# First group's sums in eight PSUM banks and two passes, its late rows from three queues, GpSimd's long products in quarters

## The reference, cut to what matters

```python
u = x * v
h = (np.maximum(pos_emb @ w1, 0) @ w2) * np.exp(-0.01 * pos)[:, None]
y = np.fft.irfft(np.fft.rfft(u, n=2 * S, axis=1) * np.fft.rfft(h, n=2 * S, axis=0), n=2 * S, axis=1)[:, :S]
a = x * y                                            # long convolution, gated
b = np.maximum(a @ w_in, 0) ** 2 @ w_out             # layer 1, 2048 hidden units
h = b @ w_in2
out = (np.maximum(h, 0) + alpha * np.minimum(h, 0)) @ w_out2   # layer 2
```

## Time and profile before

| | |
|---|---|
| median of 3 runs | 1471.96 us (1470.58 to 1472.6) |
| the profiled execution | 1473.5 us |
| its span | 1471.7 us |
| PE busy | 1451.9 us (99%) |
| DVE, ACT, POOL busy | 965.4, 799.9, 69.6 us |
| mean granted clock of PE | 0.992 |

### The profile page before, as it was taken

One profiled execution on the slowest core, in us unless ns is written; L12 is line 12 of the kernel. 1 busy time (PEld: TensorE's weight loads), 2 busy tenths in 40 slices (PEclk: granted clock), 3 DMA queues, 4 the chain that ended last, 5 costly groups with the idle time before them and its releaser, 6 DMA issues.

```text
span 1471.7 us, 18934 instructions
## 1 busy us (share of the span) xinstructions
PE 1451.9 (99%) x7106; PEld 1267.4 (86%) x7106; DVE 965.4 (66%) x1075; ACT 799.9 (54%) x1034; POOL 69.6 (5%) x51
## 2 busy tenths in 40 slices
PE   8999999799999999999999999999999999999998
PEld 8998888789888888888888888888888888888887
DVE  6876666466666666666666666666666666666664
ACT  3776677434554555455555555555555555555553
POOL 4500011121000000000000000000000000000000
PEclk9999999889999999999999999999999999999999
DMA  9545977451011011100000000000000000000000
GB/s 253 176 147 164 305 231 238 143 164 45 22 29 29 1 29 29 29 8 7 7 7 0 7 7 7 7 7 7 0 7 7 7 7 7 7 0 7 7 8 14
DMA packets 47446, 80.17 MB, mean 54 GB/s; under 512 B 4620, under 2 KB 29426, under 8 KB 46626
## 3 DMA queue, kind: packets, MB, share of 16 engines
q1 hardware_dynamic: 45170, 69.49, 15.8%
q10 hardware_dynamic: 2224, 9.98, 2.0%
HBM read 60.14 MB, written 19.23 MB: 54 GB/s over the span
## 4 chain that ended last, share of the span: by engine, by line
PE 97%; DVE 1%; ACT 1%; DMA 1%; SPq 0%; issue 0%; DVEq 0%; ACTq 0%
PE ps L172 12%; PE ps L174 12%; PE ps L161 12%; PE ps L162 12%; PE ps L173 12%; PE ps L163 12%; PE ps L627 5%; PE ps L593 4%; PE ps L672 4%; PE ps L616 3%; PE ps L608 3%; PE ps L601 1%; PE ps L576 1%; DVE g_lo L353 1%; PE ps L153 0%; PE ps L154 0%
## 5 line engine op out<-in xcount | busy, mean ns | idle before, releaser
L330 DVE SCALAR_TENSOR_TENSOR g<-ps,relu 128x960 f32<-128x960 f32 x208 | 240.7, 1157 | 199.0 <-ACT relu L278 195.9
L278 ACT ACTIVATE relu<-ps 128x960 f32<-128x960 f32 x208 | 202.6, 974 | 300.5 <-PE ps L163 300.5
L353 DVE TENSOR_TENSOR g_lo<-g,g_hi 128x960 fp32r<-128x960 f32 x208 | 245.5, 1180 | 168.7 <-ACT g_hi L291 168.6
L291 ACT CAST g_hi<-g 128x960 fp32r<-128x960 f32 x208 | 207.1, 996 | 236.1 <-DVE g L330 236.1
L172 PE MATMUL ps<-g_hi,w_hi 128*128 128x480 f32 x832 | 320.6, 385 | 3.0 <-DVE g_lo L353 2.0
L174 PE MATMUL ps<-g_lo,w_hi 128*128 128x480 f32 x832 | 319.1, 384 | 0.0
L162 PE MATMUL ps<-x_hi,w_lo 128*128 128x480 f32 x832 | 316.5, 380 | 0.0
L173 PE MATMUL ps<-g_hi,w_lo 128*128 128x480 f32 x832 | 316.3, 380 | 0.0
L161 PE MATMUL ps<-x_hi,w_hi 128*128 128x480 f32 x832 | 316.1, 380 | 0.1
L163 PE MATMUL ps<-x_lo,w_hi 128*128 128x480 f32 x832 | 313.2, 376 | 0.0
L362 DVE SCALAR_TENSOR_TENSOR g_lo<-ps,g_hi 128x960 fp32r<-128x960 f32 x208 | 239.3, 1150 | 12.9 <-ACT g_hi L298 12.9
(11 more groups left out here) (54 smaller groups left out, 1009.9 us busy)
## 6 DMA issues: line engine op xcount, KB each, us to landing
work<-dft_back SPq DMA_DIRECT2D x49, 256.0 KB, 2.9
g_dram<-work SPq DMA_DIRECT2D x49, 256.0 KB, 3.3
gt<-g_dram SPq DMA_DIRECT2D x14, 784.0 KB
gt<-x_seq SPq DMA_DIRECT2D x32, 196.0 KB
work<-v_seq SPq DMA_DIRECT2D x32, 196.0 KB
work<-dft_forward SPq DMA_DIRECT2D x49, 128.0 KB, 3.4
x<-x_gate ACTq DMA_DIRECT2D x4, 1560.0 KB, 8.1
out_t<-x SPq DMA_DIRECT2D x26, 240.0 KB, 2.0
```

The lines of the kernel that those rows point to most:

```text
L278: nc.scalar.activation(relu1[:], h[0][:, :, :T], ACT.Relu).then_inc(relu1_ready, 1)
L291: nc.scalar.copy(g_hi[0][:, s // 2 % 2], g1[:]).then_inc(g1_hi_ready, 1)
L330: nc.vector.scalar_tensor_tensor(out=g1[:], in0=h[0][:, :, :T], scalar=0.0, in1=relu1[:], op0=ALU.max, op1=ALU.mult).then_inc(g1_ready, 1)
L353: nc.vector.tensor_tensor(g_lo[0][:, s // 2 % 2], g1[:], g_hi[0][:, s // 2 % 2].bitcast(FP32), ALU.subtract).then_inc(g1_lo_ready, 1)
```

## The change

It has three parts. (1) Group 0's sums go over all eight banks, one for each of its 4 x 2 columns: a first pass over the real rows, a second over the imaginary rows, blk 1 first; the banks 7 and 6 come last in the first pass, since ACT still copies from them. The real rows of groups 0 and 1 are loaded at k = 29 and 32, the older imaginary ones at k = 42 and 43, the rest at k = 48. (2) The moves of the last two steps' rows are issued by three engines: SP takes the first half of a step (`i` = 0), ACT the second (`i` = 1), and GpSimd all four moves of step 47 for group 1, under a semaphore of their own. (3) GpSimd's three long products are cut into four pieces each, and those who wait for one now wait for four pieces.

```diff
@@ feed_forward
             if chunks[0] == 0:
-                pe.wait_ge(w_alpha_ready, 1)
+                pe.wait_ge(w_alpha_ready, F // (4 * P))
...
-                                pe.wait_ge(w3_lo_ready, 1)
+                                pe.wait_ge(w3_lo_ready, F // (4 * P))
...
         def round_0():
-            for m in range(ROUND_0):
+            sum_first_group(pe)
+            for m in range(2, ROUND_0):
                 sum_half(pe, m)
...
-                        act.wait_ge(w_scaled, 1)
+                        act.wait_ge(w_scaled, F // (4 * P))
...
-        nc.gpsimd.tensor_tensor(w_alpha.rearrange("p (c d) -> p c d", d=P),
-                                w_raw[3].rearrange("p (c d) -> p c d", d=P),
-                                alpha_sb[:].unsqueeze(2).to_broadcast([P, F // P, P]),
-                                ALU.mult).then_inc(w_alpha_ready, 1)
-        pool.wait_ge(w_alpha_ready, 1)
-        nc.gpsimd.tensor_tensor(w_raw[3], w_raw[3], w_alpha, ALU.subtract).then_inc(w_scaled, 1)
-        pool.wait_ge(w3_hi_ready, 1)
-        nc.gpsimd.tensor_tensor(w_lo[3][:], w_raw[3], w_hi[3][:].bitcast(FP32), ALU.subtract).then_inc(w3_lo_ready, 1)
+        for c in range(0, F // P, 4):
+            nc.gpsimd.tensor_tensor(w_alpha.rearrange("p (c d) -> p c d", d=P)[:, c:c + 4],
+                                    w_raw[3].rearrange("p (c d) -> p c d", d=P)[:, c:c + 4],
+                                    alpha_sb[:, c:c + 4].unsqueeze(2).to_broadcast([P, 4, P]),
+                                    ALU.mult).then_inc(w_alpha_ready, 1)
+        parts = [slice(c, c + 4 * P) for c in range(0, F, 4 * P)]
+        for n, at in enumerate(parts):
+            pool.wait_ge(w_alpha_ready, n + 1)
+            nc.gpsimd.tensor_tensor(w_raw[3][:, at], w_raw[3][:, at], w_alpha[:, at], ALU.subtract).then_inc(w_scaled, 1)
+        for n, at in enumerate(parts):
+            pool.wait_ge(w3_hi_ready, 1)
+            nc.gpsimd.tensor_tensor(w_lo[3][:, at], w_raw[3][:, at], w_hi[3][:, at].bitcast(FP32),
+                                    ALU.subtract).then_inc(w3_lo_ready, 1)
...
+        gate_half(dve, 1)
         gate_half(dve, 0)
-        gate_half(dve, 1)
         split_x1(0)
@@ long_convolution
-    def load_rows(sp, q, half, rows):
+    def load_rows(sp, q, half, rows, loaded):
...
+    moved_by_pool = sem("moved_by_pool")
+
+    def move_rows(engine, q, k, i, moved):
+
+        for part in range(2):
+            row, first = 2 * (2 * k + i) + part - R, N1 * part + GN * q
+            engine.dma_start(gt_buffers[q][row:row + 1, 1], g_sb[first:first + GN, k % 3, i]
+                             ).then_inc(moved, 16)
+
+    EARLY = K_STEPS - 8
+    early_rows = [slice(0, 2 * (2 * EARLY) - R), slice(2 * (2 * EARLY) - R, 2 * (2 * (K_STEPS - DIRECT)) - R)]
...
-                if k == EARLY + 1:
-                    stored(sp, EARLY)
-                    for q in range(2):
-                        load_rows(sp, q, 0, slice(0, R))
-                        load_rows(sp, q, 1, early_rows[0])
+                for q in range(2):
+                    if k == K_STEPS // 2 + 5 + 3 * q:
+                        stored(sp, K_STEPS // 2 + 1)
+                        load_rows(sp, q, 0, slice(0, R), half_0_loaded[q])
+                    if k == EARLY + 1 + q:
+                        stored(sp, EARLY)
+                        load_rows(sp, q, 1, early_rows[0], half_1_loaded[q])
+                sp.wait_ge(g_copied, k)
+                for q in range(k + DIRECT - K_STEPS):
+                    move_rows(sp, q, k - 1, 0, half_1_loaded[q])
                 if k == K_STEPS - DIRECT + 1:
                     stored(sp, K_STEPS - DIRECT)
                     for q in range(2):
-                        load_rows(sp, q, 1, slice(early_rows[0].stop, early_rows[1].stop))
-                sp.wait_ge(g_copied, k)
-                if k > K_STEPS - DIRECT:
-                    move_rows(sp, 0, k - 1)
+                        load_rows(sp, q, 1, early_rows[1], half_1_loaded[q])
                 sp.dma_start(g_dram[4 * k - 4:4 * k]...
...
+        pool.wait_ge(g_copied, K_STEPS - 1)
+        for i in range(2):
+            move_rows(pool, 1, K_STEPS - DIRECT, i, moved_by_pool)
...
+    def sum_first_group(pe):
+
+        def sums(banks, half):
+            for bank in banks:
+                blk, n = divmod(bank, GN)
+                if half == 0 and bank >= 6:
+                    pe.wait_ge(g_copied, K_STEPS - bank % 2)
+                last = nc.tensor.matmul(ps[:, bank, :R], gt_buffers[0][:R, half, n, blk * P:(blk + 1) * P],
+                                        idft98_sb[:R, half], start=half == 0, stop=half == 1)
+            return last
+
+        pe.wait_ge(idft98_loaded, 16)
+        pe.wait_ge(half_0_loaded[0], 16)
+        sums((0, 1, 2, 3, 4, 5, 7, 6), 0)
+        pe.wait_ge(half_1_loaded[0], 16 * (2 + 8))
+        sums(range(GN, 2 * GN), 1).then_inc(last_done, 1)
+        sums(range(GN), 1).then_inc(last_done, 1)
+
     def sum_half(pe, h):
...
-        if blk == 0 and q < 2:
-            pe.wait_ge(early_loaded[q], 16 * EARLY_DMAS)
+        if h == 2:
+            pe.wait_ge(half_0_loaded[1], 16)
+            pe.wait_ge(half_1_loaded[1], 16 * (2 + 4))
+            pe.wait_ge(moved_by_pool, 16 * 4)
...
     def gate_half(dve, h):
...
-        y = ps[:, 6 + h % 2, :GN * R].rearrange("p (n m) -> p m n", m=R)[:, :rows, :]
+        dve.wait_ge(last_done, h + 1 if h >= 2 else 2 - h)
+        if h < 2:
+            y = ps[:, GN * h:GN * (h + 1), :rows].rearrange("p n m -> p m n")
+        else:
+            y = ps[:, 6 + h % 2, :GN * R].rearrange("p (n m) -> p m n", m=R)[:, :rows, :]
...
     def scalar_program(act):      # result_copy(k)
-                move_rows(act, 1, k)
+                for q in range(k + 1 + DIRECT - K_STEPS):
+                    move_rows(act, q, k, 1, half_1_loaded[q])
```

More of the change, by code:

```diff
@@ L69, in feed_forward @@
     acc = [ps[:, 4 + k, :] for k in range(2)]
-    sum_half, gate_half, load_group, last_done, gated, w_hi_ready, w_lo_ready, alpha_loaded = last_stage
+    sum_first_group, sum_half, gate_half, load_group, last_done, gated, w_hi_ready, w_lo_ready, alpha_loaded = last_stage
     PIECES = 12
@@ L466, in long_convolution @@
     w_hi_ready, w_lo_ready = sem("w_hi_ready"), sem("w_lo_ready")
-    early_loaded = [sem(f"early_loaded{q}") for q in range(2)]
+    half_0_loaded, half_1_loaded = ([sem(f"half_{half}_loaded{q}") for q in range(2)] for half in range(2))
     gt_loaded = [sem(f"gt_loaded{b}") for b in range(3)]
@@ L481, in stored @@
             engine.wait_ge(g_stored[b], 16 * len(range(b, steps, 3)))
-    def load_rows(sp, q, half, rows):
[L485 to L497, removed]
+    def load_rows(sp, q, half, rows, loaded):
+        sp.dma_start(gt_buffers[q][rows, half], g_halves[rows, half, GN * q:GN * (q + 1), :]).then_inc(loaded, 16)
+    moved_by_pool = sem("moved_by_pool")
[6 more added lines that the diff above has]
+    early_rows = [slice(0, 2 * (2 * EARLY) - R), slice(2 * (2 * EARLY) - R, 2 * (2 * (K_STEPS - DIRECT)) - R)]
     def load_group(sp, q):
@@ L657, in tensor_program @@
                 inverse(k - 1)
+    def sum_first_group(pe):
[13 more added lines that the diff above has]
+        sums(range(GN), 1).then_inc(last_done, 1)
     def sum_half(pe, h):
         q, blk = h // 2, h % 2
-        if h == 0:
-            pe.wait_ge(g_copied, K_STEPS)
-            pe.wait_ge(idft98_loaded, 16)
         b = BUFFER[q]
-        if blk == 0 and q < 2:
-            pe.wait_ge(early_loaded[q], 16 * EARLY_DMAS)
+        if h == 2:
+            pe.wait_ge(half_0_loaded[1], 16)
+            pe.wait_ge(half_1_loaded[1], 16 * (2 + 4))
+            pe.wait_ge(moved_by_pool, 16 * 4)
         elif blk == 0:
             pe.wait_ge(gt_loaded[b], 16 * BUFFER[2:q + 1].count(b))
-        wait(pe, gated, h - 1)
+        pe.wait_ge(gated, h - 1)
         for n in range(GN):
@@ L679, in gate_half @@
         rows = size // GN
-        dve.wait_ge(last_done, h + 1)
-        if h == 0:
+        if h == 1:
             for k in range(4):
                 dve.wait_ge(gate_loaded[k], 16)
-        y = ps[:, 6 + h % 2, :GN * R].rearrange("p (n m) -> p m n", m=R)[:, :rows, :]
+        dve.wait_ge(last_done, h + 1 if h >= 2 else 2 - h)
[3 more added lines that the diff above has]
+            y = ps[:, 6 + h % 2, :GN * R].rearrange("p (n m) -> p m n", m=R)[:, :rows, :]
         x = x1[:, first:first + size].rearrange("p (m n) -> p m n", n=GN)
@@ L819, in long_convolution @@
     programs = sync_program, tensor_program, scalar_program, vector_program, gpsimd_program
-    return programs, (sum_half, gate_half, load_group, last_done, gated, w_hi_ready, w_lo_ready, alpha_loaded)
+    return programs, (sum_first_group, sum_half, gate_half, load_group, last_done, gated, w_hi_ready, w_lo_ready, alpha_loaded)
 def token_order(S):
```

## The result

The changed kernel takes 1462.49 us (median of 4 runs, 1461.83 to 1465.0), the kernel before 1472.28 (4 runs, 1470.58 to 1475.22): ratio 0.9935, 95% interval 0.9915 to 0.9954. That is 9.8 us less, inside the range of 1456 to 1466.8, but 4.5 us above the 1458 that was called likeliest, and where rival B stood (1461.6 to 1463.3). The profiled execution took 1465.0 us, its span is 1462.2.

A forecast was written before the change was run, and what follows sets the result against it. PE was taken as the bound, busy 1451.9 of 1471.7 us. Half 4 12.3 us earlier plus 2.0 of `g_lo` waits made 14.3: 1473.5 to 1459.2 profiled, median 1.5 lower, so 1458; range 1456 to 1466.8.

The forecast's parts named there:

- rival B: Clock falls in the 1.3 us idle time ahead of the second pass, 1463.3, or only after that pass, 1461.6; chance 0.24.
- A: Everything as summed, with the clock staying up through group 0's and 1's sums: 1458 us; chance 0.45.
- So I take the clock as staying up: Between the two passes PE idles 1.3 us, yet the sums behind run at full clock; half 4 12.3 us earlier.
- The moves: Last rows' moves issued by three engines: second pass can start at 282.0 instead of 285.52; bounds 281.6 and 282.9.
- GpSimd's moves: GpSimd's four moves of step 47 for group 1: done at 283, between 281.1 and 285.3; half 2 needs them at 283.9.
- C: GpSimd's moves end late, at 289; PE idles 5 us and the clock falls: 1466.8 us; chance 0.12.
- E: GpSimd's moves so late that half 2 starts later than before; at 6 us a move 1478.5 us; chance 0.03.
- Group 2: Group 2's load ahead of half 4: issued at 284.4, 4.3 us to landing at 288.7 to 289.0, in time.
- rival F: No change: PE waits for later loads, group 3 or 5 coming 12 us late; about 1470 to 1473; chance 0.04.
- Quarters: GpSimd's long products in four pieces let DVE in between, so PE's two waits for `g_lo` go: 2.0 us.
- rival D: DVE locked out by GpSimd's quarters running back to back: 1460.5 us, at worst 1465.1; chance 0.12.
- The clock's share: Of half 4's 12.3 us, the rest after 3.5 (earlier data) and 1.9 (first pass): sums and first products at full clock.

The follow-up runs named there:

- fill_sums: The changed kernel with 14 records of extra small products, result overwritten, in PE's idle time ahead of the second pass: 1458.95 us.
- no_quarters: The changed kernel with GpSimd's three long products whole again: 1463.89 us.
- store_late: The changed kernel with SP's store of step 47 put behind its moves of step 48: 1463.64 us.
- fill_half: The changed kernel with three extra small products (6 records, 0.7 us) in PE's idle time ahead of the second pass: 1461.54 us.
- fill_columns: The changed kernel with four extra wide products (256 columns), result overwritten, in PE's idle time ahead of the second pass: 1461.67 us.
- quarters_only: The kernel before with only GpSimd's three long products cut into quarters: 1470.02 us.
- before_fill: The kernel before with 15 extra wide products on PE in its 6.7 us wait for the last move: 1462.24 us.
- split_only: The changed kernel with GpSimd issuing SP's two moves for group 1 and group 2's real half loaded ahead of the last store's wait: 1462.93 us.
- old_moves: The changed kernel with moves issued as before: group 0's by SP, group 1's by ACT, none by GpSimd: 1465.75 us.

## Why the prediction was right, and where it was wrong

- The time lies inside the range, but not by the mechanism called likeliest (A, 1458). **The step that failed** is "So I take the clock as staying up". The gap was 1.9 us (1.3 was reckoned), and the clock fell at 282.84 in the trace and, by the mean granted clock (0.995 to 0.997), in all four runs. With the 13.7 us at 1.2 GHz that followed, half 4 starts 6.4 us earlier than before, not 12.3. The evidence for the step was thin: the 1.22 us stall of the earlier trace rows lay among wide layer products. Rival B had the place and the price: 1461.6 to 1463.3 against 1462.49. Its reason, though, was only half right. That small products stand on both sides of the gap is not enough: fill_sums has only small products there and keeps the clock. It takes the idle time. Both of its cases occurred: the fall ahead of the second pass (the changed kernel) and behind it (no_quarters).
- **The moves**: second pass at 3.66 us after PE's end of the middle stage (283.16 - 279.50); 3.2 was said (282.0 - 278.79), 4.1 the upper bound. The missing half microsecond is the store of step 47 ahead in SP's queue: without it store_late has 3.21. The error was not what cost the clock: fill_half has a gap of 1.2 us, about the 1.3 that was reckoned, and lost the clock in four of five runs.
- **GpSimd's moves** were bounded at 281.1 and 285.3; they hold nobody up. They were issued from 0.3 us after ACT's copy on (277.46), in 2.24 us. Rivals C and E are out. The 6 us that the Trainium skill (GPSIMD Engine Reference, section 2.1) gives for a first call of freshly loaded code do not appear.
- **Group 2**: said to be in time (landing 288.7 to 289.0 for a need at 289.0). With the clock down this was never tested in the changed kernel. With it up, PE waited 1.3 to 1.9 us. The term was mis-sized, most of all the transfer. In fill_sums it is issued 6.2 us after the end of the middle stage (284.56 - 278.36) for 5.6: the last store comes a little later, and `load_group` follows it by 2.5 us for 2.23. From issue to landing it then takes 6.14 us for the 4.3 of before:

```profile
284.56 6.14 DMA gt<-g_dram
```

In fill_columns it is 6.34 and in store_late 4.99. In the kernel before, group 2's transfer ran by itself; in fill_sums SP issues group 3's 0.4 us behind it, as the prediction said, but its sum let the two run one after the other. That they slow each other down was not tested apart. This is rival F's mechanism at an earlier place.
- **Quarters**: both waits went, as said; rival D is out: the longest `g_lo` beside quarters was 1.78 us in the changed kernel and 2.19 in quarters_only. That the 2.0 us depended on the position was missed.
- **Nothing for the rest**: right. PE's waits in the middle stage are those of before.
- **The clock's share**: predicted as 12.3 minus 3.5 and 1.9, so 6.9 us (the terms named for it in brackets add up to 6.0; the first pass's 16 records, which ran at 0.218 before, are missing among them). In before_fill, where only PE's idle time and with it the clock are changed, half 4 starts 7.9 us earlier. So the size was about right, and the changed kernel did not get it. It also shows what the old wait cost: 6.7 us of idle time, and 7.9 us for the products behind it, which ran at half speed until 301.82.

Open: at what idle time the clock falls, and when. Gaps of 1.8 and 1.9 us (no_quarters, the changed kernel) brought it down in nine of nine runs, 2.4 (split_only) in four of four, 1.2 in four of five, 0.26 and 0.72 in none of four each. A wait of 1.7 us for group 2, between wide and small products, did not in fill_sums; one of 1.9 us at the same place did in three of six runs of fill_columns. Each gap is measured in one run and taken to be alike in the others.

## What to carry to other kernels

Price a wait of TensorE with what the granted clock does after it: look at the windows behind the wait, and compare the same products' durations on both sides. If a wait can't be removed, product work in it that is thrown away can be worth as much as the whole rearrangement that shortens it (1462.24 against 1462.49 us here), and the two together more (1458.95, and 1457.36 with the shorter way to group 2's rows). When a stage gets faster, recompute the slack of the load behind it with the new times; a margin near zero is a wait, and in three of six runs of fill_columns that wait cost the clock again. Take the time of a transfer from a trace in which it runs beside the same transfers as it will: group 2's took 4.3 us in one, 6.1 in another.

## What was not expected of the hardware

- The clock fell after only 1.6 us of idle time in the changed kernel and after 3.8 in old_moves, and in fill_half 1.6 us after PE was busy again. At a gap of 1.2 us it differed from run to run of one kernel.
- Small products (98 columns) alone did not raise the clock (13.7 us of them before), but 9.3 us of them in a row kept it up.
- The start of the kernel varies: the first 128 records took 15.63 to 17.12 us, which moves everything behind them by up to 1.5 us.
- Four small DMAs issued by GpSimd took 2.24 us (0.56 each), ACT's and SP's 0.60 to 0.76 each.
